# Reordering the start of an attention, Fourier and MLP kernel: zero products, a key part in two pieces, a first maximum ahead of mask work

## The reference

```python
q_bits = (np.einsum('bhsd,dk->bhsk', q, proj) > 0).astype(np.int64)
k_bits = (np.einsum('bhsd,dk->bhsk', k, proj) > 0).astype(np.int64)
mask = q_bucket[:, :, :, None] == k_bucket[:, :, None, :]
scores = np.where(mask, scale * np.matmul(q, k.transpose(0, 1, 3, 2)), -1000000000.0)
attn = np.exp(scores - np.max(scores, axis=-1, keepdims=True))
out = np.matmul(attn / (np.sum(attn, axis=-1, keepdims=True) + 1e-09), v)
```

## Time and profile before

| What | us |
|---|---|
| Median of 3 runs | 715.86 (714.72 to 718.93) |
| The profiled execution | 714.86 |
| Its span, first to last instruction | 712.9 |
| PE busy | 703.7 (99% of the span) |
| DVE, ACT, POOL busy | 404.9, 342.8, 329.1 |

### The profile page before, as it was taken

The page is one execution under the profiler, slowest core; times in us unless marked ns, Lnnn a source line. Parts: engine busy times, 40 slices in busy tenths (PEclk is TensorE's granted clock), DMA queues, the critical chain, the costliest instruction groups (busy, mean ns, idle before and its releaser), DMA issues.

```text
span 712.9 us, 10761 instructions
## 1 busy us (share of the span) xinstructions
PE 703.7 (99%) x3746; PEld 603.5 (85%) x3746; DVE 404.9 (57%) x828; ACT 342.8 (48%) x694; POOL 329.1 (46%) x295
## 2 busy tenths in 40 slices
PE   7999999999999999999999999999999999999998
PEld 4999999999999898888888888888888888888886
DVE  7999999999999568342121221212424566745443
ACT  6999999999999664232111111111232533222111
POOL 6788888889979779553000000110043545211100
PEclk9999999999999999999999999999999999999999
DMA  6544464446332123220000001010012120000002
GB/s 185 126 127 112 120 160 117 113 119 164 92 90 79 45 59 105 86 90 17 0 1 1 0 1 45 32 49 0 1 45 89 45 67 16 1 30 16 16 30 88
DMA packets 39508, 45.97 MB, mean 64 GB/s; under 512 B 15546, under 2 KB 26936, under 8 KB 39456
## 3 DMA queue, kind: packets, MB, share of 16 engines
q1 hardware_dynamic: 36016, 41.16, 20.6%
q0 software_dynamic: 3296, 4.09, 2.5%
q10 hardware_dynamic: 144, 0.05, 0.0%
HBM read 29.23 MB, written 3.15 MB: 45 GB/s over the span
## 4 chain that ended last, share of the span: by engine, by line
PE 91%; DVE 6%; POOL 1%; issue 1%; DMA 0%; ACT 0%; POOLq 0%; DVEq 0%; ACTq 0%
PE PS L1037 21%; PE PS L1039 21%; PE PS L1038 21%; PE PS L1130 7%; PE PS L1174 4%; PE PS L1175 4%; PE PS L1193 4%; PE PS L1194 4%; DVE negmax L1424 2%; DVE ETL L1433 2%; PE PS L1285 1%; PE PS L1141 1%; PE PS L1210 1%; DVE bias L1426 0%; DMA const<-in_projb_dram 0%
## 5 line engine op out<-in xcount | busy, mean ns | idle before, releaser
L1582 DVE SCALAR_TENSOR_TENSOR HL<-PS,HH 128x512 fp32r<-128x512 f32 x48 | 33.1, 690 | 154.3 <-ACT HH L1023 154.3
L1023 ACT ACTIVATE HH<-PS 128x512 fp32r<-128x512 f32 x48 | 28.7, 598 | 182.9 <-PE PS L1039 182.9
L905 ACT ACTIVATE E<-PS,bias,factor 128x768 f32<-128x768 f32 x96 | 95.5, 995 | 12.7 <-DVE factor L1427 6.7
L1424 DVE TENSOR_REDUCE negmax<-PS 128x1 f32<-128x768 f32 x96 | 90.9, 947 | 12.3 <-PE PS L1175 12.2
L1433 DVE TENSOR_TENSOR ETL<-PS,ETH 128x384 fp32r<-128x384 f32 x192 | 97.1, 547 | 1.2 <-ACT ETH L898 1.2
L898 ACT ACTIVATE ETH<-PS 128x384 fp32r<-128x384 f32 x192 | 83.3, 488 | 1.5
L1130 PE MATMUL PS<-ident,E 128*128 128x128 f32 x576 | 79.2, 272 | 0.3
L1037 PE MATMUL PS<-UTH,W 128*128 128x512 f32 x192 | 75.7, 394 | 0.0
L1039 PE MATMUL PS<-UTH,W 128*128 128x512 f32 x192 | 74.9, 390 | 0.0
L1039 PE MATMUL PS<-W2H,HL 128*128 128x512 f32 x192 | 74.7, 389 | 0.0
L1038 PE MATMUL PS<-UTL,W 128*128 128x512 f32 x192 | 74.7, 389 | 0.0
(11 more groups left out here) (205 smaller groups left out, 1549.6 us busy)
## 6 DMA issues: line engine op xcount, KB each, us to landing
RAW<-in_moe_w_ch_dram SPq DMA_DIRECT2D x32, 256.0 KB, 2.7
QK<-in_qk_dram SPq DMA_DIRECT2D x16, 384.0 KB, 4.5
VR<-in_v_dram SPq DMA_DIRECT2D x16, 192.0 KB, 2.7
out_dram<-fin SPq DMA_DIRECT2D x12, 256.0 KB, 2.0
QM<-TOPH SPq DMA_DIRECT2D x15, 192.0 KB, 2.9
KM<-TOPL SPq DMA_DIRECT2D x15, 192.0 KB, 3.5
TOPL<-QM SPq DMA_DIRECT2D x15, 192.0 KB, 2.7
TOPH<-TOPH SPq DMA_DIRECT2D x15, 192.0 KB, 3.0
```

What stands on the lines that cost most here:

```text
L905: nc.scalar.activation(E[:, tile % NE, :], s_bank(tile)[:, 0:S], ACT.Exp, bias=bias[:, t:t + 1], scale=factor[:, t:t + 1], accum_out=esum[ ...
L1424: nc.vector.tensor_reduce(negmax[:, t:t + 1], s_bank(tile)[:, 0:S], AX_X, ALU.max, negate=True).then_inc(s_max, 1)
```

## The change

The change touches only the start.

- The zero products ahead of the projection become eight of 128 columns (there were two of 384), and the memset covers 128 columns. Behind the projection stand one zero product, two more after the key's high part, and two more after the third count of `s_first_high`.
- The key's low part comes as two instructions of POOL, of 512 and 256 columns. Tile 0's scores wait for the first, and its part of 256 keys for the second.
- POOL splits the values of head 0 ahead of its wait for `s_top`, not behind it.
- The first projection's result stands in ring banks 5 and 6, not in tile 1's pair.
- DVE makes the query's mask for columns 0 to 255 ahead of the slots. The other 512 columns follow behind the maximum of tile 0, and the low part of head 1 (second count of `s_top`) behind the maximum of tile 1. Tile 1 waits for no mask; tile 2 waits for the third count.
- The units ("bits", 1, 0) and ("bits", 1, 1) move from the slots of tiles 0 and 1 to those of tiles 2 and 3.

```diff
-        if h + 1 < NH and t == 1:
+        if h + 1 < NH and t == (1 if h else 3):
             units.append(("bits", h + 1, 1))
-        if h == 0 and t == 0:
+        if h == 0 and t == 2:
             units.append(("bits", 1, 0))
...
+        first_bits = PS[0:MW, 5:7, :].rearrange("p a b -> p (a b)")
...
-                    sp.wait_ge(s_first_key, 2)
+                    sp.wait_ge(s_first_key, 3)
...
-            nc.gpsimd.tensor_tensor(KM[0:D, 0], turned[0:D], TOPH[0:D, 0].bitcast(F32), ALU.subtract).then_inc(s_first_key, 1)
-            pool.wait_ge(s_first_key, 2)
+            for c in (slice(0, 512), slice(512, S)):
+                nc.gpsimd.tensor_tensor(KM[0:D, 0, c], turned[0:D, c], TOPH[0:D, 0, c].bitcast(F32), ALU.subtract).then_inc(s_first_key, 1)
+            pool.wait_ge(s_first_key, 3)
...
+            split_v(0)
             pool.wait_ge(s_top, 2)
-            split_v(0)
...
-            for _ in range(2):
-                nc.tensor.matmul(OT, blank[:, 0:P], blank, start=True, stop=True)
+            keep_warm(8)
...
-            nc.tensor.matmul(s_bank(1)[0:MW, 512:S], proj2[:], QK[:, 0, 512:S], start=True, stop=True).then_inc(s_first_bits, 1)
-            for _ in range(2):
-                nc.tensor.matmul(OT[:, 0:P], blank[:, 0:P], blank[:, 0:P], start=True, stop=True)
+            nc.tensor.matmul(first_bits[:, 512:S], proj2[:], QK[:, 0, 512:S], start=True, stop=True).then_inc(s_first_bits, 1)
+            keep_warm(1)
+            pe.wait_ge(s_first_key, 1)
+            keep_warm(2)
+            pe.wait_ge(s_first_high, 3)
+            keep_warm(2)
...
-                    elif tile == 1:
+                    elif tile == 2:
                         pe.wait_ge(s_first_mask, 3)
...
+                        if tile == 0 and lo:
+                            pe.wait_ge(s_first_key, 3)
...
-            first_mask(QM, 0, 0, P)
-            first_mask(QM, 0, P, S)
-            dve.wait_ge(s_top, 1)
-            nc.vector.scalar_tensor_tensor(out=TOPL[:, 1], in0=QK[:, 1], scalar=qscale[:], in1=TOPH[:, 1].bitcast(F32),
-                                           op0=ALU.mult, op1=ALU.subtract).then_inc(s_top, 1)
+            first_mask(QM, 0, 0, 2 * P)
...
+                if tile == 0:
+                    first_mask(QM, 0, 2 * P, S)
+                elif tile == 1:
+                    dve.wait_ge(s_top, 1)
+                    nc.vector.scalar_tensor_tensor(out=TOPL[:, 1], in0=QK[:, 1], scalar=qscale[:], in1=TOPH[:, 1].bitcast(F32),
+                                                   op0=ALU.mult, op1=ALU.subtract).then_inc(s_top, 1)
```

More of the change, by code:

```diff
@@ L1142, in unit, with keep_warm @@
                 last.then_inc(s_ring, 1)
-            blank = E[:, 0, 0:HC]
+            blank = E[:, 0, 0:P]
+            def keep_warm(times):
+                for _ in range(times):
+                    nc.tensor.matmul(OT[:, 0:P], blank, blank, start=True, stop=True)
             pe.wait_ge(s_blank, 1)
-            for _ in range(2):
-                nc.tensor.matmul(OT, blank[:, 0:P], blank, start=True, stop=True)
+            keep_warm(8)
             pe.wait_ge(s_proj, 1)
             pe.wait_ge(s_qk[0], 16)
-            nc.tensor.matmul(s_bank(1)[0:MW, 0:512], proj2[:], QK[:, 0, 0:512], start=True, stop=True)
-            nc.tensor.matmul(s_bank(1)[0:MW, 512:S], proj2[:], QK[:, 0, 512:S], start=True, stop=True).then_inc(s_first_bits, 1)
-            for _ in range(2):
-                nc.tensor.matmul(OT[:, 0:P], blank[:, 0:P], blank[:, 0:P], start=True, stop=True)
+            nc.tensor.matmul(first_bits[:, 0:512], proj2[:], QK[:, 0, 0:512], start=True, stop=True)
+            nc.tensor.matmul(first_bits[:, 512:S], proj2[:], QK[:, 0, 512:S], start=True, stop=True).then_inc(s_first_bits, 1)
[4 more added lines that the diff above has]
+            keep_warm(2)
             for tile, et, pv, us in slots:
@@ L1402, in update @@
                 nc.vector.tensor_tensor(upper, upper, DS[:, t, ::-1, 1:LH], ALU.add).then_inc(s_u, 1)
-            nc.vector.memset(E[:, 0, 0:HC], 0.0).then_inc(s_blank, 1)
+            nc.vector.memset(E[:, 0, 0:P], 0.0).then_inc(s_blank, 1)
             dve.wait_ge(s_first_high, 1)
@@ L1410, in first_mask @@
             def first_mask(to, row, lo, hi):
-                nc.vector.tensor_scalar(to[D:D + NM, 0, lo:hi], s_bank(1)[row:row + NM, lo:hi], gamma[row:row + NM, 0:1],
+                nc.vector.tensor_scalar(to[D:D + NM, 0, lo:hi], first_bits[row:row + NM, lo:hi], gamma[row:row + NM, 0:1],
                                         gamma[row:row + NM, 1:2], ALU.is_gt, ALU.mult).then_inc(s_first_mask, 1)
             first_mask(KM, KROW, 0, S)
-            first_mask(QM, 0, 0, P)
-            first_mask(QM, 0, P, S)
-            dve.wait_ge(s_top, 1)
-            nc.vector.scalar_tensor_tensor(out=TOPL[:, 1], in0=QK[:, 1], scalar=qscale[:], in1=TOPH[:, 1].bitcast(F32),
-                                           op0=ALU.mult, op1=ALU.subtract).then_inc(s_top, 1)
+            first_mask(QM, 0, 0, 2 * P)
             for slot, (tile, et, pv, us) in enumerate(slots):
```

## The result

The changed kernel takes 718.08 us (median of 22 runs, 717.21 to 718.72), the kernel before 715.63 (22 runs, 714.72 to 718.93). The ratio is 1.0029, with a 95% interval from 1.0022 to 1.0036: 2.1 us slower, clear of noise and within the half per cent that was forecast as no change. The medians themselves lie 2.45 us apart. The forecast was 716.8 in a range from 714.3 to 719.4. The profiled execution took 717.42, its span 715.0 us; before, 714.86 and 712.9.

What follows compares the result with a forecast made beforehand. DVE's chain was taken to bound the start until 18.9 us. Its terms, -0.33 + 0.77 + 0.94 = +1.38 us, took the profiled 714.86 to 716.2; half of a 1.0 us median difference made 716.8, range 714.3 to 719.4.

Steps and rivals of the forecast that it cites:

- The frame: Start: DVE's unbroken chain sets the pace to 18.9 us; the shift built up by about 19.5 is carried to the end.
- Rival A: Start: the first maximum's head start counts and the moved work hides; -0.3 us, 715.5; chance 0.1.
- The moved work: DVE behind the first maximum: mask's 512 columns (+0.77 us) and low part of head 1 (+0.94 us) lengthen the chain.
- the sum: DVE's chain +1.4 us, tile 6 +0, zero products inside it: profiled execution from 714.86 to 716.2, median 716.8.
- the first maximum's gain: Tile 0's maximum on DVE starts 0.33 us earlier, at 9.13 in place of 9.46.
- The key's pieces: POOL's low part of the key: 512 columns take 1.26 us and 256 take 0.73, ending at 7.75 and 8.5.
- I take 4.65: Projection's start on PE behind the eight zero products: 4.65 us, 0.15 later than before; bounds 0 and 0.8.
- rival D: Zero products delay the projection by the full 0.8 us, lag 1.9, 717.4; forecast together with this case: chance 0.6.
- Rival C: Some executions start at 1.2 GHz around the first scores; zero products end that, median about 715.9; chance 0.12.
- Tile 6's cover: Margin between the last mask move's landing (21.3 to 22.1) and tile 6's scores (22.06): 0 to 0.8 us, no stall.
- Rival B: Tile 6 waits for its mask move, PE stands 0.3 to 1.3 us, 717.5; chance 0.15.
- Adding half of the difference to the median of three runs: The three-run median lay 1.0 us above the profiled execution; half of that was added to 716.2, giving 716.8.

Runs made afterwards that it cites:

- The order alone: The kernel before with only DVE's new order, the moved bits units and the first projection in ring banks; ratio 1.0024, median 717.63 us.
- the changed kernel's second profile: The changed kernel, unchanged, profiled once more: span 715.7 us, key's mask at 6.20, sixth maximum at 21.71.
- products in the gap: The changed kernel with ten more products of 384 columns on PE between the scores of tiles 1 and 2; ratio 1.0025, median 717.97 us.
- no front zeros: The kernel before without any zero product ahead of the projection; ratio 1.0037, median 718.19 us.
- the run with both edits: The changed kernel with the query's other 512 mask columns ahead of the first maximum and ten products between tiles 1 and 2; ratio 1.0016, median 717.80 us.

## Why the prediction was right, and where its size was off

**The frame held.** The shift at about 19.5 us is carried to the end: tile 6's score starts 2.06 us later than before, the span is 2.1 longer. The chain runs through DVE and goes over to PE at 20.88, where 20.3 was forecast. Rival A is out, since the sixth maximum starts at 21.20 and not by 19.5.

**The moved work held.** It was +0.77 + 0.94 on DVE's chain with the first maximum as its zero. Measured from the first to the sixth maximum, the changed kernel takes 11.77 us and before 9.81, so +1.96. By the starts of the maxima, 0.96 of it is the mask's 512 columns, where the sum had 0.77 (from the first to the second maximum it is 2.13 us, before 1.76 with a mask read of 0.59 in it); 0.94 is the low part, as forecast; the rest, 0.06, is what moving the two mask reads changed. The order alone, in the kernel before, gives the same 14.54 us from mask to sixth maximum.

**The term that was mis-sized is the first maximum's gain**, -0.33 in the sum and -0.03 in the profiled execution. The key's pieces were even cheaper than assumed (1.27 and 0.71 us, over at 8.3), but they no longer decided. The step that failed is "I take 4.65" with "the full clock reached by 4.5, as before": the zero products held PE until 4.75, and the clock rose during the projection. Masks started at 6.65, not 6.28, and the first score waited for the mask. That is rival D, which had the mask 0.65 us later than the sum; it came 0.37 later. The moment of the rise differs from execution to execution, as the lengths of the two 512-column projection records show: 1.05 us in all in the changed kernel's second profile, 1.94 with products in the gap. The zero products ahead are the same in both, and that edit lies behind the projection.

**Not in the sum: the clock in the new gap.** The prediction had PE's gap between the scores of tiles 1 and 2 (scores there at 9.8, the next at about 11.5) and gave it no price, since DVE was the bound. That holds in one execution (0.1 us at most, by the products in the gap) and not in another (0.8 us, 12.59 less 11.77). Rival C had looked for the clock at the first scores, where the change puts its zero products, and expected a gain from it. It was right that the kernel before has executions with a lower clock, some 2 us longer (24 of 82), and wrong that the change ends them: the change opens a gap right behind its zero products, and the clock is low in all 22 of its executions. The 718.93 that it leaned on need not come from the start, since the one profiled execution with such an excess (721.95, no front zeros) has it at 284 us.

**Tile 6's cover** was forecast at 0 to 0.8 us. The last mask move was issued at 20.12 (forecast: 19.5 to 20.3), and tile 6's score came 0.12 us behind where PE was ready, at 22.72. It started 2.6 us behind that issue, and 3.0 with the mask first and the products in the gap, where I had read 1.7 to 1.8 from head 2's traffic. That reading was too short. Either the wait ends later than the bytes, or the bytes came later here, beside the next moves that SP had issued by then (21.66 and 22.24 in the run with both edits); the runs don't tell which. The Trainium skill, "DMA: Bandwidth & Descriptors", section "Anatomy of one DMA", gives about 2.0 us of fixed cost for the GpSimd path; from the start of the issue on SP's queue, the traces show more than that. Rival B was there, at 0.1 us (only the run with both edits shows the wait put down to the DMA), and 0.5 where DVE's chain was made shorter.

**The sum against the profiled execution.** 716.2 was forecast and 717.42 measured. Nearly all of the 1.2 us is accounted for: the first maximum (0.30), the mask of 512 columns (0.19), the mask reads (0.06), tile 6 (0.13) and 0.46 us around the span (2.42 us against 1.96). The sum had no term for the last. That the result still fell into the range owes something to luck: its upper part had been made for rival B's stall, which came at a tenth of a us.

**The median.** That 2.45 us between the medians, 2.1 by the ratio and 2.1 of span in the profiles look alike is partly chance. Between the medians there are some 1.65 us of span and 0.64 around it, by the second table; the profiled execution of before was one of its quickest. Adding half of the difference to the median of three runs was a guess that helped nothing, since 22 runs put the median of before at 715.63.

**What stays open.** Three things: why kernels with more zero products take 0.6 to 1.0 us more around the span; where the clock falls in the 24 low-clock executions of before; and how the moment at which the clock rises is set, since the key's mask starts anywhere from 6.2 to 7.6 us in the profiles with eight narrow zero products in front. The fallen clock's own share of the loss is small in the median: 0.1 us between the changed kernel and the one with products in the gap, less than the noise.

## What to carry to other kernels

Where the profile shows one engine without a gap from the start to the point at which the bound engine takes over, reordering that engine's work to serve the first tile sooner wins at most the head start, and every instruction put behind it is lost if a hole opens ahead of it. Look for the hole first: if the first result can't come before the engine is through with its preparations, leave them where they are. Price a new gap on the matmul engine with the clock in it, and ask how much of the slow stretch behind it the bound engine can cover.

## What the runs showed of the hardware

- The granted clock in the profile reads 1.00 over the first microseconds, while matmuls there run at the lower level, 1.2 GHz: 1.94 us for two 512-column float32 records in one execution and 1.05 in another of the same front. Without front zero products the records stay long (0.63 us in place of 0.39) up to about 13.6 us, and the clock still reads 1.00. Only record lengths show the rise.
- After it had risen, the clock fell to 0.50 around a gap of 1.86 us in PE's work: in one execution just behind it (low from a little past 12 to 15.6), in the other within it (from about 11 to 17.7). It did not fall around the 1.73 us of idle time before. With ten products in the gap it stayed at 1.00.
- A DVE instruction with two inputs in SBUF, 128 x 768, takes 1.63 us beside a POOL subtraction and 1.02 without it. The Trainium skill, "GPSIMD Engine Reference", section "Specifications", has GpSimd's interfaces to SBUF shared with VectorE for such instructions; the two runs agree.
